# Expert layer of an attention, mixture-of-experts and MLP kernel: one weight load issued from another queue, one register load placed elsewhere

## What is computed

```python
logits = x @ w_gate                      # x: 768 x 512, w_gate: 512 x 8
expert_idx = np.argmax(logits, axis=1)
...
h = np.maximum(np.einsum('ecd,edf->ecf', disp, w1), 0.0)   # w1: 8 x 512 x 1024
y = np.einsum('ecf,efd->ecd', h, w2)                       # w2: 8 x 1024 x 512
...
out[i] = gate_w[i] * y[expert_idx[i], pos[i]]
```

## Time and profile before

| | us |
|---|---|
| median of 3 runs | 412.69 (412.60 to 412.78) |
| the profiled execution, its own time | 412.77 |
| its span, first to last instruction | 411.0 |
| TensorE busy | 397.0 |
| first layer of the experts, L714, matmuls | 60.0 |
| second layer of the experts, L730, matmuls | 59.2 |

### The profile page before, as it was taken

One profiled execution on the slowest core, in us unless ns is written; L12 is line 12 of the kernel. 1 busy time (PEld: TensorE's weight loads), 2 busy tenths in 40 slices (PEclk: granted clock), 3 DMA queues, 4 the chain that ended last, 5 costly groups with the idle time before them and its releaser, 6 DMA issues.

```text
span 411.0 us, 7244 instructions
## 1 busy us (share of the span) xinstructions
PE 397.0 (97%) x2666; PEld 365.1 (89%) x2668; DVE 249.9 (61%) x442; ACT 200.3 (49%) x388; POOL 81.4 (20%) x81
## 2 busy tenths in 40 slices
PE   8899999999999899899999999999999999999995
PEld 3688898898999789799999999999988999899984
DVE  5888989989989541201101111118899998877761
ACT  5968968968778220210110110117667555553441
POOL 1910320320600050474534600000000000000005
PEclk9999999999999999999999999999999999999999
DMA  8856913972600055999899999900000000000003
GB/s 299 268 119 186 233 21 81 306 164 66 218 2 0 8 203 176 425 410 337 306 349 348 362 347 382 332 9 0 2 0 0 2 2 2 0 0 2 0 2 153
DMA packets 15451, 62.85 MB, mean 153 GB/s; under 512 B 2112, under 2 KB 2752, under 8 KB 11328
## 3 DMA queue, kind: packets, MB, share of 16 engines
q1 hardware_dynamic: 14032, 58.51, 42.2%
q0 software_dynamic: 960, 3.15, 2.0%
q10 hardware_dynamic: 432, 0.83, 0.5%
HBM read 49.89 MB, written 3.15 MB: 129 GB/s over the span
## 4 chain that ended last, share of the span: by engine, by line
PE 51%; DMA 4%; DVE 4%; ACT 2%; issue 1%; POOL 1%; POOLq 0%; SPq 0%; DVEq 0%
PE ps L814 14%; PE ps L714 13%; PE ps L730 12%; PE ps L789 12%; DMA ring<-in_w 2%; DMA rows<-xg,sloti 1%; DVE nt__120 L1310 1%; ACT lt L1024 1%; DVE nt__120 L1293 1%; ACT at__119 L1027 1%; DVE hn L1315 1%; DVE hn L1308 1%; ACT et L1012 0%; POOL rows L457 0%; DVE at__119 L1290 0%
## 5 line engine op out<-in xcount | busy, mean ns | idle before, releaser
L714 PE MATMUL ps<-xs,ring 128*128 x512 | 60.0, 278 | 1.6 <-DMA ring<-in_w 1.2
L714 PEld LDWEIGHTS ps<-xs,ring 128*128 128x128 f32 x512 | 58.5, 191 | 3.0 <-issue 3.0
L730 PE MATMUL ps<-hs,ring 128*128 128x128 f32 (+1 forms) x512 | 59.2, 276 | 0.0
L730 PEld LDWEIGHTS ps<-hs,ring 128*128 128x128 f32 x512 | 58.5, 192 | 0.0
L1172 DVE TENSOR_TENSOR ptl<-ps,pth 128x384 fp32r<-128x384 f32 x96 | 48.8, 550 | 4.3 <-ACT pth L937 4.2
L937 ACT ACTIVATE pth<-ps 128x384 fp32r<-128x384 f32 x96 | 42.2, 495 | 18.6 <-PE ps L648 18.0
L1115 DVE TENSOR_REDUCE nmax<-ps 128x1 f32<-128x768 f32 x48 | 45.7, 955 | 4.2 <-PE ps L534 2.6
L534 PE MATMUL ps<-ops 128*128 128x384 f32 x192 | 44.4, 352 | 1.4 <-ACT prob L899 1.4
L899 ACT ACTIVATE prob<-ps,nmax 128x768 f32<-128x768 f32 x48 | 43.5, 907 | 1.7 <-DVE nmax L1115 1.6
L789 PE MATMUL ps<-yh,wih 128*128 128x384 f32 x128 | 43.1, 336 | 0.3 <-ACT hc L1016 0.3
L648 PE MATMUL ps<-cfs,prob 128*128 128x128 f32 x288 | 41.3, 276 | 1.8 <-DVE ptl L1172 1.5
(11 more groups left out here) (160 smaller groups left out, 677.5 us busy)
## 6 DMA issues: line engine op xcount, KB each, us to landing
ring<-in_w SPq DMA_DIRECT2D x32, 1024.0 KB, 7.7
winraw<-in_w_in SPq DMA_DIRECT2D x8, 512.0 KB, 7.6
woutraw<-in_w_out SPq DMA_DIRECT2D x8, 512.0 KB, 8.7
ops<-kh SPq DMA_DIRECT2D x12, 192.0 KB, 3.4
ops<-qh SPq DMA_DIRECT2D x6, 384.0 KB, 5.7
xg<-rows SPq DMA_DIRECT2D x1, 1539.0 KB, 7.2
raw<-in_vt SPq DMA_DIRECT2D x4, 384.0 KB, 5.1
raw<-in_qt SPq DMA_DIRECT2D x3, 384.0 KB, 6.7
```

The lines of the kernel that those rows point to most:

```text
L714: last = mm(ps[:, fc // 2, (fc % 2) * WIDE:(fc % 2) * WIDE + W], wa[:, 2 * fc // KF, kd, P * (fc % (KF // 2)):P * (fc % (KF // 2)) + P], x ...
L730: last = mm(ps[:, 4 + half * KD // 2 + k, 0:W], wb[:, half, fc, P * k:P * k + P], hs[:, fc, 0:W], start=(fc == 0), stop=(fc == KF - 1))
```

## The change

It has two parts. First, `wa` half 0 of the second expert (expert 1) is issued by ACT instead of SP: inside the first expert's window, after ACT's first ReLU, ACT waits for `Hw` 2 and issues the DMA on its own queue. SP skips that load in its first pass and goes straight to half 1. Second, PE no longer loads `bounds` at the top of the loop. Expert 0's values are loaded before the loop into two fixed registers; the top of the loop copies these two into `st` and `n_e`; and the values of expert e+1 are loaded between the first and the second half of the second layer of expert e. `bounds` gets a ninth row for the load in the last pass.

```diff
--- before.py
+++ after.py
...
-        bounds = place("bounds", [P, E, 2], I32)
+        bounds = place("bounds", [P, E + 1, 2], I32)
...
@@ -284,6 +284,11 @@
+
+        def first_half_weights(engine, e, half):
+
+            engine.dma_start(wa[:, half, :, :], w1[bass.ds(e, 1), half, :, :, :].rearrange(
+                "o p c n -> (o p) c n")).then_inc(s[f"wa{half}"], 16)
 
...
@@ -347,8 +352,7 @@
             def first_weights(e, half):
-                sp.dma_start(wa[:, half, :, :], w1[bass.ds(e, 1), half, :, :, :].rearrange(
-                    "o p c n -> (o p) c n")).then_inc(s[f"wa{half}"], 16)
+                first_half_weights(sp, e, half)
 
...
@@ -383,9 +387,11 @@
             sp.dma_start(xg[:, :, :], rows.rearrange("(t p) x -> p t x", p=P)).then_inc(s["back"], 16)
 
             with sp.Fori(0, E - 1) as i:
-                for half in range(2):
-                    hold(sp, s["passed_sp"], s["Hw"], 4 * i + 2 * half + 2)
-                    first_weights(i + 1, half)
+                with sp.If(i > 0):
+                    hold(sp, s["passed_sp"], s["Hw"], 4 * i + 2)
+                    first_weights(i + 1, 0)
+                hold(sp, s["passed_sp"], s["Hw"], 4 * i + 4)
+                first_weights(i + 1, 1)
                 hold(sp, s["passed_sp"], s["Yc"], i + 1)
                 second_weights(i + 1, 0)
                 hold(sp, s["passed_sp"], s["Yw"], i + 1)
...
@@ -701,8 +707,10 @@
+            at_r, many_r = pe.alloc_register("expert_start"), pe.alloc_register("expert_count")
+            pe.reg_load([at_r, many_r], bounds[0:1, 0, :])
             with pe.Fori(0, E) as e:
-                st, n_e = load_bounds(pe, e)
+                st, n_e = (pe.snap(x, min_val=0, max_val=T) for x in (at_r, many_r))
 
                 def window(W):
...
@@ -721,6 +729,8 @@
                         pe.wait_ge(s["ya"], 2 * e + half + 1)
                         pe.wait_ge(s["yd"], 2 * e + half + 1)
                         pe.wait_ge(s[f"wb{half}"], 16 * (e + 1))
+                        if half:
+                            pe.reg_load([at_r, many_r], bounds[0:1, bass.ds(e + 1, 1), :].rearrange("p a b -> p (a b)"))
                         for fc in range(KF):
                             if half == 0 and fc % 4 == 0:
                                 pe.wait_ge(s["Ha"], 2 + 2 * e + fc // 4 + 1)
...
@@ -966,6 +976,10 @@
                         av(hs[:, 2 * b:2 * b + 2, 0:W],
                            ps[:, b, 0:2 * WIDE].rearrange("p (a c) -> p a c", a=2)[:, :, 0:W],
                            ACT.Relu).then_inc(s["Ha"], 1)
+                        if b == 0:
+                            with act.If(e < 1):
+                                hold(act, s["passed_act"], s["Hw"], 2)
+                                first_half_weights(act, 1, 0)
                     for half in range(2):
                         ks = slice(half * KD // 2, (half + 1) * KD // 2)
...
@@ -1229,8 +1243,8 @@
-            V.tensor_copy(bounds[:, :, 0], ps[:, 2, 0:E])
-            V.tensor_copy(bounds[:, :, 1], ps[:, 2, E:2 * E]).then_inc(s["bnd"], 1)
+            V.tensor_copy(bounds[:, 0:E, 0], ps[:, 2, 0:E])
+            V.tensor_copy(bounds[:, 0:E, 1], ps[:, 2, E:2 * E]).then_inc(s["bnd"], 1)
```

More of the change, by code:

```diff
@@ L216, in attention_moe_mish @@
         sems = {}
-        for n in ["first_" + n for n in MISH_A + MISH_B] + ["still", "c0", "c", "cr", "k0", "q0", "k1", "q1", "pj", "pj2", "passed_sp", "passed_gp", "rk0", "rk1", "rv0", "rv1", "ca", "cq", "cp", "pja", "pjb", "ah", "ab", "ao", "ak", "aq", "ka", "kl", "ks", "ch", "cc", "opsA", "opsB", "wa0", "wa1", "wb0", "wb1", "Yc", "wi", "wo", "out",
+        for n in ["first_" + n for n in MISH_A + MISH_B] + ["still", "c0", "c", "cr", "k0", "q0", "k1", "q1", "pj", "pj2", "passed_sp", "passed_act", "passed_gp", "rk0", "rk1", "rv0", "rv1", "ca", "cq", "cp", "pja", "pjb", "ah", "ab", "ao", "ak", "aq", "ka", "kl", "ks", "ch", "cc", "opsA", "opsB", "wa0", "wa1", "wb0", "wb1", "Yc", "wi", "wo", "out",
                   "pjh", "pjl", "wg",
```

## The result

The changed kernel took 414.47 us (median of 8 runs, 412.36 to 416.60), the kernel before 412.54 beside it: a ratio of 1.0050 [1.0033, 1.0068]. 410.8 was forecast. The kernel is slower, by 0.5%, and the time is outside the range. So the result has two parts to explain: why nothing is gained, and why the first eight runs lost as much as 2 us.

A forecast was written before the change was run, and what follows sets the result against it. PE was taken as the bound, busy 397.0 of 411.0 us. Gains of 0.4 (early weights), 0.45, 0, 0.15 and 0.87 (register load) sum to 1.87, taking the median from 412.69 to 410.8, range 410.1 to 412.5.

The forecast's parts named there:

- The register load: Tops of later experts: moving the load gains 0.45 at expert 2, 0.15 at expert 4, 0.87 at experts 5 to 7.
- the step on the landing of its weights: Expert 4: `wa0` lands at 214.7, a tenth before PE's sequencer asks, so it gains 0.15, not 0.28.
- the lead of 2.0 us: Second layer: PE's sequencer is 2.0 us ahead of the array, so the moved load of about 0.65 costs zero.
- (a): Experts 4 to 7: the weight stream becomes the bound, leaving a gain of 1.02, 411.7; chance 0.14.
- (b): Later experts' tops: sequencer time does not cause the short losses, so only part one's 0.4 stays, 412.3; chance 0.10.
- The wait for expert 1's weights: Before expert 1's first layer: 1.25 us idle ended by weights; the early DMA removes this, copies into `xs` come next.
- the term of 1.0: Before expert 1's first layer: about 1.0 of the 1.25 us idle can go, before contention is subtracted.
- The release of the DMA: Inside expert 0: `Hw` 2 comes half way between two ReLUs, at 154.6, and ACT's DMA leaves at about 154.8.
- d: Scatter's tail and everything serial behind it: delay by the early weights, taken as 0.6, with ends 0 and 2.8.
- (d): Scatter's tail: as (c), plus the code-fetching engine finishing last, delay 3.8, 414.0; chance 0.06.
- (c): Scatter's tail: the whole 1 MB goes ahead of it, delay 2.8, 413.0; chance 0.10.

The follow-up runs named there:

- e1: Changed kernel with half 0 of expert 1's `wa` given back to SP, so the register load alone: 410.00 us, 0.9959 of the kernel before.
- e14: The register load alone against the kernel before, measured again on another chip: 410.01 us, ratio 0.9970.
- e12: The kernel before, unchanged, profiled again: 411.58 us in its one run.
- e9: The changed kernel, unchanged, measured again on another chip: 411.76 us, 1.0004 of the kernel before.
- e6: Register load kept; SP issues expert 1's weights at 143.9 into a spare tile, POOL copies them into the ring: 409.92 us, 0.9960 of the kernel before.
- e5: The kernel before, unchanged, profiled again: 412.20 us.
- e8: Changed kernel, but ACT issues the early weights only after the scatters have landed: 413.90 us, 1.0045 of the kernel before.
- e2: Changed kernel with bounds loaded at the top of each pass, so ACT's DMA alone: 413.41 us, 1.0040 of the kernel before.
- e13: The changed kernel, unchanged, measured again on another chip: 411.61 us, 1.0013 of the kernel before.
- e15: ACT's DMA alone against the kernel before, measured again on another chip: 413.58 us, ratio 1.0062.
- e4: Changed kernel with ACT moving only 0.5 MB early, SP the other half later: 411.32 us, 0.9999 of the kernel before; profiled execution 416.52.
- e7: e6 with the load into the spare tile issued by ACT at 150.5: 416.53 us, 1.0109 of the kernel before.
- e11: Changed kernel with SP issuing the early weights at `Hw` 2, before its wait for the scatters, ACT nothing: 411.73 us, 1.0004 of the kernel before.

## Why the prediction was wrong, point by point

**The register load: right.** Forecast 1.47 us; e1 gained 1.5 and e14 1.4. In the profiles the stretch from expert 1 to the Mish stage went from 103.52 (e12) to 101.89 (e1), 1.63, both without a wait at expert 1. Experts 2 and 4 each gained the full loss (7.84 and 7.14 in the chain of after, no issue), where I had kept back 0.07 and 0.13. For expert 4 the step on the landing of its weights was too careful. The load between the halves took 0.54 of PE's sequencer, and no issue appeared in any second layer, so the lead of 2.0 us did cover it (group of the line in after: min/median/max ns, first and last start):

```profile
L733 PEldq TENSOR_LOAD <-bounds x8: 536/539/558, 160.2 to 271.4; - x8
```

Rivals (a), 411.7 by a weight stream that bounds, and (b), 412.3 by a cause other than the sequencer, fall with e1 and e14.

**The wait for expert 1's weights: there, but not always.** It is gone in every profile with the early DMA, and the copies into `xs` are next, as forecast: e9's first layer of expert 1 is 0.89 for six records, 0.05 of issue and 6.74. But the term of 1.0 was read from one execution. e12 shows none of it, so over many executions the term is smaller.

**The release of the DMA: 154.8 was forecast, 156.25 measured.** I took `Hw` 2 half way between two ReLUs. ACT's timeline in the changed kernel:

```profile
154.66 0.38 ACT L976 ACTIVATE hs<-ps 128x256 f32<-128x256 f32 x1 [3.62 <-remote]
156.25 0.34 ACTq L290 DMA_DIRECT2D ring<-in_w  x1
156.72 0.38 ACT L976 ACTIVATE hs<-ps 128x256 f32<-128x256 f32 x1 [1.68 <-PE ps L722]
```

The first ReLU starts at 154.66 and not near 152.84. PE itself was on time. All nine profiles in which ACT or SP waits there for `Hw` 2 show the DMA leaving 5.2 to 5.4 us after expert 0's start, where 4.0 was forecast. In e6 POOL waits for the same `Hw` 2, and its copy starts 4.0 after expert 0, at 155.57. And e12, the unchanged kernel, has its ReLUs late too:

```profile
156.53 0.81 ACT L966 ACTIVATE hs<-ps 128x256 f32<-128x256 f32 x2 [5.13 <-PE ps L714]
```

So the added wait is not the only cause. Of the six profiles without it in which ACT's first ReLU can be seen, three have it 2.1 after expert 0 (before, e5, e8) and three at 3.6 to 5.2 (e14, e1, e12); of the nine with it, all have it at 3.6 or later. Whether the wait makes the late case more frequent, and why the signals of PE arrive late at all, stays open.

**d, the step that failed.** I bounded contention against the tail of the scatter only, from 0 to 2.8 us (3.8 in (d)), and wrote that everything behind it would be delayed by d. The scatter landed 5.39 after its issue in the profile, 0.76 more than before (d = 0.6 was taken), and 3.90 in e9, within what the kernel before shows (e12: 3.6, e5: 4.8). What I never priced, and so put at nothing, was the read-back behind it: in the first profile it took 2.8 more, so the path was delayed by 3.5 and not by 0.6. I left it out because by my times the 1 MB, started at 155.8 and moved in 2.8, was through at 158.6, just as the read-back was issued. Both numbers were wrong. Table by stretch of after:

```profile
156.50:157.50 1.00, 1.00 (x11) 1.00 0.29 25
157.50:159.00 1.50, 1.50 (x16) 1.00 1.00 169
159.00:160.50 1.50, 1.50 (x16) 1.00 0.79 273
160.50:162.00 1.50, 1.50 (x16) 1.00 0.98 325
```

The first bytes come at 157.4 and not at 155.8, and for 1.5 us they move 169 GB/s with the engines full, against 346 in the stream whose rate I had used (32.93 MB in 95 us). Then the queues of after, in 159.5 to 161 and in 161 to 162.5:

```profile
q10 hardware_dynamic: 61, 0.50, 85.1%
...
q1 hardware_dynamic: 133, 0.27, 72.2%
q10 hardware_dynamic: 35, 0.16, 28.2%
q8 instruction: 1, 0.02, 4.0%
```

The read-back (q1) was issued at 159.46 and has no packet before 161: it waits until most engines are through with the weights, and lands 9.98 after its issue instead of 7.2. The Trainium skill's rule ("DMA: Bandwidth & Descriptors", "Queues, rings and completion order"), an engine takes whole packets of a queue in turn, agrees with these rows, as far as totals over 16 engines can show it: q10 has 85% and q1 nothing, until most of the weights are through. In the prediction I had weighed this rule against the scatter, the transfer that it hardly touched.

How much this late start explains differs. In the kernel before, the first packets of the read-back come 1.1 us after its issue. In e9 they come 2.9 after it (issued 157.89, none before 160.75), and this start, 1.8 later than before, covers the 1.6 that e9's read-back takes longer. In the profile of the changed kernel they come 1.6 after it, so the start explains 0.5 of the 2.8. The rest is a tail. The queues of after in 162.2 to 164, and all packets in 166.5 to 168.7:

```profile
q10 hardware_dynamic: 4, 0.02, 4.9%
...
DMA packets 164, 0.95 MB, mean 430 GB/s; under 512 B 15, under 2 KB 15, under 8 KB 61
```

Four of the weights' packets trail here, where e9 has none after 161.4, and 61 - 15 = 46 of the read-back's 768 pieces of 2052 bytes move only after 166.5, where e9 has none left. The landing, at 169.44, waits for the last of them. That few engines were held up, and the others not, fits this; why they were is not shown. The code fetch (q8) came at 157 before and at 161.4 here; in e9 it came at 157 with the weights moving, so it is not shown that they hold it.

The added time of the read-back, against 7.2 (7.6 in e12), is 2.8 us in the first profile, 2.0 in e2, 1.6 to 1.7 in e9, e13 and e15. It makes PE idle 2.26 us before the transposes in e2 and 2.02 in e15, where e12 has none, and that is about the 2.0 and 2.2 us that ACT's DMA costs alone; the expert stage behind it is the same (103.43 and 103.45, against 103.52). Rivals (c) and (d) forecast 413.0 and 414.0, near the first measurement, but by a mechanism that did not occur: the 1 MB did not go ahead of the scatter's tail.

**No term for the clock.** My sum priced idle time of PE at its length. Over the profiles of both kernels and of all edits without a filler: after 3.76 us or more of idle (4.04 after, 3.76 e4, 4.54 e7, 4.44 e8) the transposes ran at 0.50 and took 5.35 to 5.38; after 2.26 or less (e2 2.26, e15 2.02, e9 1.42, e13 1.39, e11 1.22, the longest of before 0.82) at 1.00, in 2.84 or less. So the profiles with the long gaps pay 2.5 us more for the clock, and the others nothing. The first eight runs of the changed kernel show it: 412.36 with a mean clock of 0.999, the other seven 414.02 to 416.60 with 0.990 to 0.995. In e9 and e13 three of 24 runs were at 0.994 or 0.995 (413.31 to 414.29), the others near 411.6. The kernel before is not free of it: beside e1, two of its 25 runs had a mean clock of 0.994 (413.25 and 413.97). So the two measurements differ, as far as the profiles tell, in how often the gap was one of the long ones; why it was so often in the first is not shown.

**What settles the account.** By the runs: register load -1.4 to -1.5, ACT's DMA +2.0 to +2.2. With both, +0.2 in two measurements, where both intervals include no difference, and +1.9 in the first. The 0.6 us between the sum of the parts and the whole on e13's chip lie within e15's interval (1.0 us to either side). The best version has the register load alone (410.0), and it beats both kernels. Staging the weights early (e6, 409.92) adds nothing to it: in both chains expert 1 begins with six matmuls in 0.89 and an issue of 0.05, as in e12's, so not the weights but the copies into `xs` are last there.

## What to carry to other kernels

Before a transfer is moved earlier, list every transfer in flight until it has landed, the one issued after it included, and give its start and its rate in that place, not in a full stream: here a prefetch of 1 MB, worth 1.0 us at best, delayed a 1.5 MB transfer on the critical path by 1.2 to 2.8. Its mean rate doesn't give its end, which waits for its last pieces: 46 of 768 were late in the worst profile. Ask how long the gap in front of TensorE may become, since a long one lets its clock fall and costs more than its length. And see whether a wait stands in several executions before a gain is counted for it; taking work off a sequencer just ahead of its engine's next block gave what its rows said.

## What the runs showed of the hardware

- The granted clock fell to 0.50 in all four profiles with 3.76 us or more between PE's blocks and in none with 2.26 or less; in after it was 0.50 from 169.5 to about 175.
- A new 1 MB load from HBM moved 169 GB/s in its first 1.5 us with all engines shown as busy, then 273 and 325. The read-back of e12, too, began slower: 104 GB/s at a share of 0.58 in 158.8 to 160.5, then 301.
- A busy DMA share says nothing of who is served: 85% for q10, and the transfer on the critical path had none of it. Of the read-back's 768 pieces 46 moved after 166.5 in after, none in e9.
- PE's first signals of expert 0 reached ACT late in some executions of either kernel, with PE's own records on time: ACT's first ReLU started 2.1 us after expert 0 in one profile of the kernel before, 5.2 in another (152.84 and 156.53), 3.6 in after. POOL's copy in e6, released by a later signal, started 4.0 after expert 0.
